# Top-k attention in front of an MLP and a switch layer: the select of VectorE becomes a mask, an add on GpSimd and an exponential in place

## The reference

```python
scores = scale * np.matmul(q, k.transpose(0, 1, 3, 2))   # 4 x 8 heads, 576 rows, 64 wide
kth = np.partition(scores, -top_k, axis=-1)[..., -top_k:-top_k + 1]   # top_k = 32
scores = np.where(scores >= kth, scores, -1000000000.0)
scores = scores - np.max(scores, axis=-1, keepdims=True)
attn = np.exp(scores)
attn = attn / (np.sum(attn, axis=-1, keepdims=True) + 1e-09)
out = np.matmul(attn, v)
# then 2304 tokens: h = x @ w_in (512 -> 2048); g = max(h, 0) + alpha * min(h, 0); x = g @ w_out
# then the switch layer: gate, one of 8 experts per token, x + gate * relu(x @ w1) @ w2
```

## Time and profile before

| | us |
|---|---|
| median of 3 runs | 1219.06 (1214.24 to 1221.98) |
| the profiled execution | 1216.73, its span 1215.0 |
| VectorE busy | 958.9 (79%) |
| TensorE busy | 946.3 (78%) |
| ScalarE busy | 588.2 (48%) |
| GpSimd busy | 422.0 (35%) |

### The profile page before, as it was taken

How to read it: one execution, slowest core, us unless ns; L and a number is a source line. 1 busy time by engine, 2 the same in 40 slices (tenths; PEclk the granted TensorE clock), 3 DMA queues, 4 the chain that set the end, 5 groups by cost and what they waited for, 6 DMA issues and landing times.

```text
span 1215.0 us, 21163 instructions
## 1 busy us (share of the span) xinstructions
PE 946.3 (78%) x6064; PEld 626.0 (52%) x6065; DVE 958.9 (79%) x2112; ACT 588.2 (48%) x1234; POOL 422.0 (35%) x553
## 2 busy tenths in 40 slices
PE   4345556447899889889888978998898998399895
PEld 2223323225665657556665756666576776144342
DVE  5999999999999999999999999999974800411111
ACT  2345444436844873684587368458636911011000
POOL 2122353653821671383176138317610000101010
PEclk9957565658997999999999999999898999599998
DMA  9224121301002100300200030020014451434640
GB/s 282 91 94 142 35 85 49 96 3 31 2 11 63 26 10 1 88 0 10 69 20 10 2 86 0 10 69 2 1 33 149 140 169 50 162 129 149 212 138 18
DMA packets 72615, 83.09 MB, mean 68 GB/s; under 512 B 47164, under 2 KB 51260, under 8 KB 70976
## 3 DMA queue, kind: packets, MB, share of 16 engines
q1 hardware_dynamic: 67120, 57.19, 15.8%
q0 software_dynamic: 5392, 24.65, 5.8%
HBM read 71.59 MB, written 11.53 MB: 68 GB/s over the span
## 4 chain that ended last, share of the span: by engine, by line
DVE 30%; issue 29%; PE 28%; DMA 5%; ACT 3%; DVEq 2%; POOL 2%; SPq 0%; POOLq 0%; ACTq 0%
DVE best L948 9%; DVE arena L961 8%; DVE arena L969 8%; PE acc L538 7%; PE acc L525 5%; PE sc L642 3%; DMA arena<-in_moe_w_dram 3%; PE pt_full L709 2%; PE sc L477 2%; DVEq L20 2%; PE pt_full L495 2%; DVE row_den L978 1%; PE acc L506 1%; DMA arena<-in_v_dram 1%; PE pt_full L717 1%
## 5 line engine op out<-in xcount | busy, mean ns | idle before, releaser
L948 DVE MAX8 best<-arena 128x8 f32<-128x576 f32 x576 | 403.4, 742 | 5.7 <-ACT arena L766 3.2
L961 DVE MATCH_REPLACE8 arena<-best,arena 128x576 f32<-128x576 f32 x432 | 315.8, 738 | 0.0
L1232 POOL TENSOR_SCALAR arena<-arena,row_inv 128x576 f32<-128x576 f32 x144 | 105.4, 747 | 351.7 <-DVE row_inv L981 351.6
L525 PE MATMUL acc<-arena 128*128 (+1 forms) x1536 | 203.2, 289 | 26.5 <-ACT neg_part L812 19.4
L495 PE MATMUL pt_full<-ident,arena 128*128 128x128 f32 x576 | 108.8, 320 | 140.6 <-POOL arena L1232 86.3
L538 PE MATMUL acc<-arena 128*128 128x288 f16 x1472 | 200.8, 289 | 0.0
L525 PEld LDWEIGHTS acc<-arena 128*128 128x128 f16 x1536 | 147.7, 98 | 77.8 <-issue 34.5
L495 PEld LDWEIGHTS pt_full<-ident,arena 128*128 128x128 f32 x576 | 75.9, 162 | 180.9 <-issue 96.7
L538 PEld LDWEIGHTS acc<-arena 128*128 128x128 f16 x1472 | 143.7, 99 | 43.7 <-issue 8.2
L969 DVE SCALAR_TENSOR_TENSOR arena<-arena,best 128x576 f32<-128x576 f32 x144 | 142.1, 1033 | 1.9 <-ACT arena L773 1.9
L766 ACT ACTIVATE arena<-sc 128x576 f32<-128x576 f32 x144 | 92.2, 643 | 104.7 <-PE sc L477 87.2
(11 more groups left out here) (160 smaller groups left out, 1030.1 us busy)
## 6 DMA issues: line engine op xcount, KB each, us to landing
arena<-in_moe_w_dram SPq DMA_DIRECT2D x64, 512.0 KB
arena<-in_moe_w_in_dram POOLq DMA_DIRECT2D x8, 1024.0 KB, 5.9
arena<-in_moe_w_out_dram POOLq DMA_DIRECT2D x8, 1024.0 KB, 5.8
arena<-in_v_dram POOLq DMA_DIRECT2D x4, 1152.0 KB, 6.1
x_rows<-x2n SPq DMA_DIRECT2D x24, 192.0 KB, 2.5
out_dram<-x2n SPq DMA_DIRECT2D x24, 192.0 KB, 2.7
nat<-in_q_dram SPq DMA_DIRECT2D x32, 128.0 KB, 2.4
nat<-in_k_dram SPq DMA_DIRECT2D x32, 128.0 KB, 2.7
```

The lines of the kernel that those rows point to most:

```text
L525: last = nc.tensor.matmul(dst[:, 0:HALF], win16[:, a, d, f * P:(f + 1) * P], xT16[:, bass.ds(row + d, 1), b, bass.ds(col, HALF)].rearrange ...
L948: nc.vector.max(best[:, gp, j, r, :], src).then_inc(max_found if r == 0 else dve_step, 1)
L961: nc.vector.match_replace(left[:, j, :], best[:, gp, j, r, :], src, MASKED).then_inc(dve_step, 1)
L1232: nc.gpsimd.tensor_scalar(probs[:, gp, j, :], probs[:, gp, j, :], row_inv[:, gp, j:j + 1], 1.0, ALU.mult, ALU.mult)\
```

## The change

The selection no longer waits for the exponential. VectorE's three selects become three `tensor_scalar` instructions that write 0 or -1e30 into `probs` (is less than the 32nd, times -1e30). GpSimd (`drop`) adds the scores to them. ScalarE takes the exponential of `probs` in place and sums the rows with its accumulator. `invert` moves from the first round of the next search to its third and waits for ScalarE. `exps` stands behind the second tile of a group (`EXP_AFTER = 1`) instead of the first; for the group at the head of a pair also behind the second, where it was behind the third. `store_scores` waits for the add instead of the inverse. The `leak` columns are laid out anew, in two parts around each `normalise`, and TensorE's `down` waits for the columns of each part alone.

```diff
@@ store_scores, exps (ScalarE) @@
-                if not (isinstance(p, int) and p == 0):
-                    act.wait_ge(inv_ready, GROUPS * (p - 1) + g + 1)
                 for t in [GROUP * g + j for j in js]:
                     n = TILES * p + t
+                    if not (isinstance(p, int) and p == 0):
+                        act.wait_ge(masked, n - TILES + 1)
...
-                    nc.scalar.activation(probs[:, gp, j, :], scores[:, GROUP * g + j, :], ACT.Exp,
-                                         bias=neg_max[:, gp, j:j + 1], scale=SCALE).then_inc(exp_ready, 1)
+                    act.wait_ge(masked, TILES * p + GROUP * g + j + 1)
+                    nc.scalar.activation(probs[:, gp, j, :], probs[:, gp, j, :], ACT.Exp, bias=neg_max[:, gp, j:j + 1], scale=SCALE,
+                                         accum_out=row_sum[:, gp, j:j + 1]).then_inc(exp_ready, 1)
@@ search, invert (VectorE) @@
-                        elif j < 2 and not first:
-                            invert(GROUPS * p + g - 1, 1 - gp, steps.base + steps.used, j)
+                        if r == 2 and j < 2 and not first:
+                            invert(GROUPS * p + g - 1, 1 - gp, j)
...
+                n = GROUPS * p + g
+                if not isinstance(n, int) or n >= 2:
+                    hold(dve, pt_ready, GROUP * (n - 1))
                 for j in range(GROUP):
-                    hold(dve, dve_step, steps.base + steps.used - GROUP + 1)
-                    hold(dve, exp_ready, TILES * p + GROUP * g + j + 1)
-                    nc.vector.scalar_tensor_tensor(out=probs[:, gp, j, :], in0=tiles[j], scalar=best[:, gp, j, ROUNDS - 1, 7:8],
-                                                   in1=probs[:, gp, j, :], op0=ALU.is_ge, op1=ALU.mult,
-                                                   accum_out=row_sum[:, gp, j:j + 1]).then_inc(dve_step, 1)
-                    steps.used += 1
+                    hold(dve, dve_step, steps.base + steps.used - GROUP + j + 1)
+                    nc.vector.tensor_scalar(probs[:, gp, j, :], tiles[j], best[:, gp, j, ROUNDS - 1, 7:8], OUTSIDE, ALU.is_lt, ALU.mult)\
+                        .then_inc(mask_ready, 1)
...
-                    hold(dve, dve_step, masked)
+                    hold(dve, exp_ready, GROUP * (n + 1))
@@ GpSimd @@
+            def drop(p, par, g):
+                gp = (GROUPS * par + g) % 2
+                for j in range(GROUP):
+                    t = GROUP * g + j
+                    hold(pool, mask_ready, TILES * p + t + 1)
+                    nc.gpsimd.tensor_tensor(probs[:, gp, j, :], scores[:, t, :], probs[:, gp, j, :], ALU.add).then_inc(masked, 1)
...
+                        drop(2 * i + par, par, g)
                         for n in split_slots.get(slot, ()):
                             split(n)
                         normalise(2 * i + par, par, g)
...
-            leak_parts = {(0, 0): range(0, 5), (0, 1): range(5, 12), (0, 2): range(12, FT1)}
+            leak_parts = {(0, 1): (range(0, 2), range(2, 5)), (0, 2): (range(5, 9), range(9, 12)), (1, 0): (range(12, 14), range(14, FT1))}
...
+                        drop(2 * i + par, par, g)
+                        parts = leak_parts.get((par, g), ((), ()))
+                        leak(pool, nc.gpsimd, i - MLP_LAG, parts[0])
                         normalise(2 * i + par, par, g)
                         if g == 0:
                             low_x(2 * i + par - 1)
-                        leak(pool, nc.gpsimd, i - MLP_LAG, leak_parts.get((par, g), ()))
+                        leak(pool, nc.gpsimd, i - MLP_LAG, parts[1])
@@ down (TensorE) @@
-                    if d == 0:
-                        hold(pe, g_ready, NEG + FT1 * (m + 1))
                     items.open = begin(items)
+                if d == 0:
+                    hold(pe, g_ready, NEG + FT1 * m + fs[-1] + 1)
```

17 lines of the change are left out of this document (11 added, 6 removed).

## The result

The changed kernel takes 1380.2 us (1373.06 to 1380.84, four runs), the kernel before 1218.8 us beside it: a ratio of 1.133, 95% interval 1.128 to 1.138. The forecast was slower, at 1322 us with 1365 as the upper end, so the sign was right and the size was not: 163 us more in the profiled executions, where I had counted 105.

The account below looks back on a forecast made before the run. VectorE was taken to set the pace at 105.9 us a step. A longer chain of waits would make it 120.9, +90 us over six steps, with +15 before the loop: 1216.7 + 90 + 15 = 1322 us, range 1256 to 1365.

Parts of the forecast that it names:

- The walk of the step: One loop step followed through its chain of waits across the engines: 120.9 us instead of 105.9, +15.0 a step.
- the ring of four: Up half, four buffers: exponentials of (0, 2) wait behind ScalarE's column 12, which needs GpSimd's column 8; four columns 8.9 us.
- the adds of (0, 2): Up half, GpSimd: three adds, 4.2 us, begin only after columns 2 to 4, though the masks were ready earlier.
- The port's cost: VectorE and GpSimd take turns: a 1.4 us add between the masks makes a search 17.3 us instead of 15.9.
- the close of the maxima: Ahead of the loop, VectorE's close waits for loads, exponentials and sums: about 8.5 us instead of 1.6, +7.
- rival E: Waits slow TensorE's clock in the loop: 8 us a step more, 1370 us; chance 0.12.
- Before the loop: Twelve searches with three longer chains and costlier masks, less savings in split searches: +15 us, bounds 0 and +25.
- VectorE's waits at the inverse: In the loop, VectorE waits for ScalarE's exponentials some 17 us a step, longest in the search of (1, 0), 7 to 11.
- C: Adds overlap masks and exponentials end by 9.2 us into each search; TensorE decides: -24 us, 1193 us; chance 0.05.
- A: Likeliest case: the step's longer chain and the cost before the loop as forecast, 1322 us (1290 to 1355); chance 0.66.
- B: The buffer ring binds only for (0, 2), nothing carried to the next pair: step 109.8 us, 1256 us; chance 0.13.
- D: Only the shared port matters, every third mask waiting for an add: 103.8 us a step, 1219 us; chance 0.04.

Follow-up runs that it names:

- e9_warm1: e1_short with ten more transposes of 128 columns on TensorE ahead of each wait for a pair's probabilities: 1335.2 us.
- e1_short: The changed kernel without ScalarE's waits for the add in `store_scores`, which shortens its loop body: 1370.9 us.
- e5_short_exp0: e1_short with the exponentials behind the first tile of a group instead of the second: 1294.2 us.
- e10_inv2: e5_short_exp0 with the inverse in the second round of the next search instead of the third: 1283.7 us.

## Why the prediction was right in sign and wrong in size

What held. VectorE ceased to be the bound, and a longer way from search to transpose became it. The walk of the step closed through the places I had named: exponentials behind the second tile, the ring of four, the adds of (0, 2) behind column 4, TensorE in the down half. With the clock up and the pauses gone (e9_warm1) the step measured 121.5 us against 120.9, and each piece is right within 0.7 us. The port's cost, the add and the mask were sized right, as was the close of the maxima.

What failed are three terms that the sum put at nothing: TensorE at its lower clock, ScalarE's pauses, and, ahead of the loop, the way from VectorE to PV. They are worth about 36, 9 and 15 us, and 163 exceeds 105 by 58. In the middle of the loop the step measured 131.9 us, forecast 120.9:
- **The exclusion of rival E** (TensorE's lower clock). I took PV's 5.5 us and the columns from rows at 0.98 and made the lower clock a case of its own, with a chance of 0.12. It is no alternative to the walk: the walk produces the idle time that lowers the clock. Its own price was 8 us a step, and e9_warm1 against e1_short measured 8.2, 36 us in all. That the two agree is in part luck: the price spread 15% over 54 us, and 5.2 of the 8.2 us sit in the two PV alone. Where I went wrong is the reading of the earlier trace rows as a rule of busy shares over a stage: e5_short_exp0 has PV at 7.2 to 8.1 us with TensorE 87% busy. The walk also contained the gap of 3.3 us ahead of PV, in which work brought the clock back. My own sign for E, a clock under 0.9 in the loop, came: 0.88. Its 1370 us was the nearest of my figures to 1380.
- **ScalarE's pauses**, 2.2 us a step, not foreseen: nothing in the profile of before shows them, since that kernel has none.
- Small: an exponential that also sums takes 0.76 us from start to start instead of 0.66, 0.2 us or so in each group of three.
- **Before the loop**, +15 was forecast for VectorE and 11.5 came, but PV comes 30.1 later. The sum had only VectorE's delay. The rest is the longer way from the start of the search to PV (29.9 us for 11.3): 11 us for the inverse's place, some 5 for GpSimd's splits that now end after it, and the exponentials ahead of the third tile. This is read from the trace; no run took the three apart. The 15.7 us of e10_inv2 do not show it, since nearly all of them are VectorE's.
- VectorE's waits at the inverse: 28.9 us in the step shown where about 17 were forecast, the longest (10.3) in the search of (0, 2), not of (1, 0), which has 9.3. The rise is the step's, since 132.7 - 28.9 = 103.8 us, VectorE's own work, is what it was said to be.
- A slip that decided nothing: C's 1193 leaves out the +15 before the loop that A, B and D carry; with it C is 1208.

Rivals B, C and D are out: no step came near 110, 102 or 106 us while the inverse was late and the exponentials stood behind the tiles. What C hoped for, VectorE's saving, was 37 us on the selections and 18 us of VectorE's busy time in all.

What the 163 us are made of, read from the runs one after another: the pauses 9 (1380.2 to 1370.9), the exponentials behind the second tile 77 (to 1294.2), the adds 52 (to 1242.3), and 25 are left for the late inverse less what the masks save (to 1217). The order in which parts are taken away matters: the adds are worth 29 us with the exponentials behind the second tile and 52 with them behind the first. How the 77 divide can be read from the four runs with and without the clock's edit: with it the exponentials' place is still worth 61.5 us (1335.2 to 1273.7), so the queue is the larger part and the clock some 15. A ring of more than four buffers, which would test that link alone, has no room in the memory of this kernel and was not tried.

## What to carry to other kernels

When a step joins a circle of engines, its place in the queue of each engine costs more than its length: here 2.3 us of exponentials, one tile earlier or later, moved the time by 77 us, and a late inverse cost 42 or 209 us depending on whether the exponentials stood ahead of the tiles or behind one. Walk the new circle as done here, then look in the walk for new waits of TensorE ahead of long matmuls and price these matmuls at the lower clock too, as a part of the sum and not as a rival to it. Where a long GpSimd instruction shares a port with VectorE, move the moment at which its input arrives, so that it falls beside instructions that it doesn't hold; that was the only gain on the kernel before (1.2%), and it came from a run that seemed to show nothing.
